# Loading the first piece of a weight in two halves, and one product of zeros fewer ahead of it

## What is computed

```python
# attention: for each token t
y[:, :, t] = einsum('bhd,bhde->bhe', rt, state + u*kt (x) vt)
state = w * state + kt (x) vt
# first feed-forward part: x (3072, 384), w1 and w2 (384, 1024), w3 (1024, 1024), w_out (1024, 384)
a = x @ w1
b = x @ w2
h = a * b @ w3
x = h @ w_out
# second: w_in (384, 2048), w_out (2048, 384)
h = x @ w_in
out = (h * cos(h)) @ w_out
```

## Time and profile before

| | us |
|---|---|
| median of 3 runs (lowest to highest) | 791.63 (791.34 to 792.43) |
| the profiled execution's own time | 792.66 |
| its span, from the first to the last record | 791.2 |
| TensorE busy, matmuls | 784.6 (99%) |
| VectorE busy | 429.4 (54%) |
| ScalarE busy | 376.4 (48%) |
| GpSimd busy | 345.8 (44%) |

### The profile page before, as it was taken

One profiled execution on the slowest core, in us unless ns is written; L12 is line 12 of the kernel. 1 busy time (PEld: TensorE's weight loads), 2 busy tenths in 40 slices (PEclk: granted clock), 3 DMA queues, 4 the chain that ended last, 5 costly groups with the idle time before them and its releaser, 6 DMA issues.

```text
span 791.2 us, 15799 instructions
## 1 busy us (share of the span) xinstructions
PE 784.6 (99%) x6500; PEld 677.2 (86%) x6500; DVE 429.4 (54%) x639; ACT 376.4 (48%) x647; POOL 345.8 (44%) x279
## 2 busy tenths in 40 slices
PE   8999999999999999999999999999999999999998
PEld 6999999888999888998888888888888888888886
DVE  7998655543644433123289555546555554554553
ACT  4634222222222222224367667656665765665664
POOL 2646766556566553111234335334333432433432
PEclk9999999999999999999999999999999999999999
DMA  8775445342344320202221010000001001001001
GB/s 335 267 244 149 114 145 152 91 137 85 105 139 144 89 88 22 80 0 73 68 80 41 2 41 0 1 8 33 1 1 40 1 1 40 1 1 39 2 1 40
DMA packets 47595, 57.32 MB, mean 72 GB/s; under 512 B 21794, under 2 KB 34211, under 8 KB 47523
## 3 DMA queue, kind: packets, MB, share of 16 engines
q1 hardware_dynamic: 34898, 45.83, 17.9%
q10 hardware_dynamic: 12624, 10.49, 4.3%
HBM read 46.86 MB, written 9.44 MB: 71 GB/s over the span
## 4 chain that ended last, share of the span: by engine, by line
PE 96%; DVE 3%; issue 1%; ACT 0%; POOL 0%; DVEq 0%; POOLq 0%
PE p_h L1164 25%; PE p_acc L1164 13%; PE p_a L1164 13%; PE p_b L1164 13%; PE p_out L1385 8%; PE p_out L1381 8%; PE p_out L1382 8%; PE p_s L1188 2%; PE p_y L1200 1%; PE p_y L1204 1%; PE p_acc L1313 1%; PE p_kv L1192 1%; DVE w3t_l L982 1%; PE p_b L1320 0%; PE p_acc L1299 0%
## 5 line engine op out<-in xcount | busy, mean ns | idle before, releaser
L626 POOL TENSOR_TENSOR g_l<-g,g_h 128x512 fp32r<-128x512 f32 x96 | 149.9, 1561 | 241.6 <-ACT g_h L814 241.6
L1113 DVE TENSOR_TENSOR g<-angle,p_h 128x512 f32<-128x512 f32 x96 | 65.8, 686 | 109.1 <-ACT angle L823 109.1
L490 POOL TENSOR_TENSOR g_l<-g,g_h 128x384 fp32r<-128x384 f32 (+1 forms) x56 | 70.2, 1253 | 121.0 <-ACT g_h L663 121.0
L1381 PE MATMUL p_out<-g_h,wq_l 128*128 128x512 f32 x288 | 112.1, 389 | 0.0
L1164 PE MATMUL p_h<-y_l,wi_h 128*128 128x512 f32 x288 | 112.1, 389 | 0.0
L1164 PE MATMUL p_h<-y_h,wi_h 128*128 128x512 f32 x288 | 112.1, 389 | 0.0
L1164 PE MATMUL p_h<-y_h,wi_l 128*128 128x512 f32 x288 | 112.1, 389 | 0.0
L1382 PE MATMUL p_out<-g_h,wq_h 128*128 128x512 f32 x288 | 112.0, 389 | 0.0
L814 ACT CAST g_h<-g 128x512 fp32r<-128x512 f32 x96 | 59.7, 621 | 67.5 <-PE p_out L1385 42.3
L658 ACT COPY g<-p_a 128x384 f32<-128x384 f32 (+1 forms) x56 | 29.4, 526 | 119.1 <-PE p_a L1164 117.5
L819 ACT ACTIVATE angle<-angle 128x512 f32<-128x512 f32 x96 | 60.6, 631 | 49.6 <-DVE angle L1123 49.6
(11 more groups left out here) (118 smaller groups left out, 1642.2 us busy)
## 6 DMA issues: line engine op xcount, KB each, us to landing
krT_raw<-in_kr_dims SPq DMA_DIRECT2D x24, 512.0 KB, 4.1
kr_raw<-in_kr_tokens SPq DMA_DIRECT2D x24, 384.0 KB, 4.7
v_raw<-in_v_tokens SPq DMA_DIRECT2D x24, 192.0 KB, 4.8
x_raw<-y_transposed SPq DMA_DIRECT2D x24, 192.0 KB, 2.5
out<-out_sb SPq DMA_DIRECT2D x17, 256.0 KB, 2.0
stage_b<-in_moe_w_in SPq DMA_DIRECT2D x8, 384.0 KB, 3.1
stage_b<-in_moe_w_out SPq DMA_DIRECT2D x8, 384.0 KB, 3.0
y_transposed<-yT ACTq DMA_DIRECT2D x24, 96.0 KB, 2.6
```

The costliest lines, as they stand in the source:

```text
L490: nc.gpsimd.tensor_tensor(g1_l[:, n % 2, cols], g1[:, n % 2, cols], g1_h[:, n % 2, cols].bitcast(F32), ALU.subtract).then_inc(s_gl, 1)
L626: nc.gpsimd.tensor_tensor(g2_l[:, par, :], g2[:, par, :], g2_h[:, par, :].bitcast(F32), ALU.subtract).then_inc(s_g2l, 1)
L1113: nc.vector.tensor_tensor(g2[:, n % 2, :], angle[:, n % 2, :], p_h[n % 4][:, :], ALU.mult).then_inc(s_g2, 1)
L1381: mm(bank[t][:, :], wq_l[:, f, cols], g2_h[:, f % 2, :], start=f == 0, stop=False)
```

## The change

`WARM` goes from 4 to 3. The load of the first piece of w_out becomes two transfers of 128 rows (192 KB) each: the first signals a new semaphore `s_row0`, the second the piece's old one, `s_st[0]`. Both are issued where the one was, so ScalarE's queue has one transfer more to issue. TensorE's product (0, 0) waits for `s_row0` alone, product (0, 1) for `s_st[0]`; ScalarE's copy of the first piece waits for both. The same bytes are loaded to the same place, and no product of real operands is added or taken away.

```diff
-WARM = 4
+WARM = 3
...
+    s_row0 = sem("first_128_rows_of_w_out_loaded")
...
+        def start_first_piece():
+
+            place = staged(A_SLOTS, 0, wo_st[0])
+            act.dma_start(place[:, 0, :], wo_st[0][:, 0, :]).then_inc(s_row0, 16)
+            act.dma_start(place[:, 1, :], wo_st[0][:, 1, :]).then_inc(s_st[0], 16)
+
         def piece(i):
 
             act.wait_ge(s_st[i % 4], 16 * (i // 4 + 1))
+            if i == 0:
+                act.wait_ge(s_row0, 16)
...
         start_w3_half(0, 0)
-        start_piece(0)
+        start_first_piece()
         start_w3_half(1, 0)
...
-            if t % 2 == 0:
+            if t == 0:
+                pe.wait_ge(s_row0, 16)
+            elif t == 1 or t % 2 == 0:
                 pe.wait_ge(s_st[t // 2], 16)
```

## The result

| | before | after |
|---|---|---|
| median of 20 executions (lowest to highest), us | 792.17 (791.34 to 793.43) | 794.22 (791.88 to 796.40) |
| ratio after / before | | 1.0022 [1.0014, 1.003] |
| the profiled execution, its span, us | 792.66, 791.2 | 794.52, 793.0 |

The kernel became slower: the medians are 2.05 us apart, and the ratio, an estimate of its own and not the quotient of the medians, says 0.22%, which is 1.7 us (the forecast was 0.34 us faster). Its executions scatter over 4.5 us where those of before scatter over 2.1. Five of the 20 took 792.4 us or less, as long as before. The profiled one is a typical one. Of 93 executions of before timed later, beside the experiments, 92 lie between 790.91 and 794.30 us, and one, with a granted clock of 0.56, took 1313.74.

A forecast was written before the change was run, and what follows sets the result against it. The prediction took TensorE's queue, with little waiting, as the bound. Its sum was -0.335 us at the fifth record, +0 issue, +0 waits, -0 lost behind: 791.63 - 0.34 = 791.3 us, range 790.2 to 792.8.

The forecast's parts named there:

- Three products of zeros, the first 128 rows on their own: TensorE's head: zeros end at 4.79 us, first half lands at 4.64, first real product starts at 4.98 instead of 5.65.
- late half: Rival at the first piece's load: both halves land together at about 5.3 us; 791.6 us, chance 0.10.
- postponed rise: Rival at TensorE's head: a pause after the zeros delays the clock's rise to 10.10 us; 792.7 us mostly, chance 0.12.
- What the low clock is worth: TensorE's head: starting 0.67 us earlier at the low clock gains half of that, 0.335 us.
- The second half, and the queue that issues it: ScalarE's queue: the added issue delays later transfers 0.47 us but costs nothing; shorter runs cost 0 to 0.1 us.
- +0 for the issue: Term of the sum for the added transfer issue on ScalarE's queue: no cost; without cover, 0.47 us.
- Where the gain goes behind the head: VectorE's chain after the head: the 0.335 us gain passes tile 2's landing and line 898, so nothing is lost.
- Swallowed: Rival behind the head: first 17 us run 0.34 us faster but VectorE's chain doesn't move; 791.6 us, chance 0.18.

The follow-up runs named there:

- e4: The kernel before, with SP waiting for the second half of w3's tile 0 instead of piece 1, so released later; 793.03 us, ratio 1.0008.
- e9: The kernel before, with the keys' chunk 1 loaded ahead of its transposed form on SP's queue; 792.38 us, ratio 1.0001.
- e11: The kernel before, no transfer added, with ScalarE's issues from the third on held for 0.7 us; 792.71 us, ratio 1.0005.
- e1: The kernel before with three products of zeros instead of four, the first piece still whole; 792.29 us, ratio 0.9999.
- e6: The kernel before with one more transfer, of 4 KB, in second place on ScalarE's queue; 792.76 us, ratio 1.0007.
- e3: The kernel after, with SP waiting for the first half of w3's tile 1 instead of piece 1; 792.35 us, ratio 1.0003.
- e8: The kernel after, with the keys' chunk 1 loaded ahead of its transposed form on SP's queue; 793.20 us, ratio 1.0013.
- e2: The kernel after with four products of zeros again, the first piece still in two halves; 792.98 us, ratio 1.0012.

## Why the prediction was wrong

**Three products of zeros, the first 128 rows on their own: right, and too cautious.** The zeros ended at 4.79 as computed. The first half landed at the lower end given, 4.47, so the first product started at 4.79 and not 4.98, and there was no gap. The late half and the postponed rise did not occur.

**What the low clock is worth: right rule, and a size that hung on the moment of the rise.** The advance was 0.86 us, half of it 0.43; the clock rose at 6.75 instead of 7.19, and half of those 0.44 us are 0.22 more. Together they are the 0.65 us at the fifth record. The ninth record (8.36 us) then waited for piece 1, landed at 8.31, and lost 0.12, which leaves 0.53 at the third piece (11.48 against 12.01) where 0.335 was forecast. The 0.22 can't be credited to the change: the moment of the rise moves by 1 us between before, e4 and e9, with the same TensorE work.

**"The second half, and the queue that issues it": this step failed.** It is the term "+0 for the issue" of the sum. It put the added issue at nothing and the shorter runs at 0 to 0.1 us, and argued that the landing of piece 1's neighbour hangs on bytes and not on the issue. Measured were 1.17 us on piece 1. By e11 a late issue alone is worth 0.47 at most, about what e1 shows without one, and in e6's one trace 4 KB more went with over a microsecond. The bytes were the same; that a transfer more changes how the others run was in no row of before. Worse, the step listed who waits for piece 1 on TensorE, and used SP's issue at 7.16 merely as a clock for the landing. SP's wait on that piece, with the attention's loads and tiles 2 and 3 behind it, was never priced. The cover of piece 1 was given as the ninth record at 8.65; on SP it was zero. e3, which moves that wait to an earlier landing, takes the loss away; it releases SP at 6.01, so it removes more than the 1.17 us.

**"Where the gain goes behind the head": right places, wrong sign.** The step named tile 2's landing with 0.3 us of cover and line 898 with 0.47, and asked whether a gain would pass. Both covers hang on SP's queue. Turned the other way they are what a delay of over 1 us runs into: 0.7 us at line 982 (17.54 to 18.26), then line 898. "Swallowed" was a rival without loss; the loss through the same two places should have been the rival on the slower side, in place of the postponed rise. e1 is the swallowed case itself: the first burst of attention products 0.5 us earlier (16.76 against 17.27), median unchanged.

**The base.** The forecast of 791.3 us stands on the median of three executions, 791.63; that of twenty is 792.17. This 0.54 us of error is the sample's and not the mechanism's. From 792.17 the same sum gives 791.8 us, still faster than before where after is slower.

**How the 2.36 us at tile 7 divide.** Only in part. The head's gain doesn't count against it: ScalarE took the first sum at 15.55 instead of 16.08 and then waited 1.15 us for tile 2. VectorE was 0.72 us behind at line 991, 1.31 at `rT_sc` ahead of line 907, and 2.27 at line 907, so the wait for GpSimd's product is the last 0.96 of it. The late release of SP alone accounts for some 0.5 by e4. The rest goes with transfers that land later than in e4 although SP issued the first of them at the same time: tile 2 (17.16 against 16.30) and the keys' chunk 1, at 22.2 us, where e4 and e6, with SP as late, had it at 19.73 and 19.85. Of that chunk's 16 parts 14 had landed by 20.16 us, the last two at 21.80 and 22.16. A fetch of instructions of 16 KB ran from 20.71 to 21.67; it can't be the reason everywhere, since in e3, where the last part of the chunk landed at 21.06 and the others by 19.47, the fetch began at 20.79 and was still running. That this lateness matters is made likely by e8, whose interval overlaps that of after; that it comes in some executions and not in others fits the five fast ones of after; what decides it stays open. e3's chunk was late with SP early, so it isn't SP's lateness alone. The difference between after (1.0022) and e2 (1.0012) is not settled either.

## What to carry to other kernels

Before adding a transfer to a queue, list every wait on every engine that hangs on the transfers issued after it, those of the queues that issue other loads first, and price each by its own slack. When a gain is bounded by some cover behind it, ask also what happens if that place comes later: the same cover bounds the loss. And time many executions: here the loss shows as scatter as much as in the median.

## What the runs showed of the hardware

A transfer more among the first few, of 192 KB or of 4 KB, went with a landing some 1 us late at unchanged bytes (plus 4 KB in e6), in seven of eight profiles. The longest packet of 1.5 to 3 KB between 3 and 9 us took 0.87 to 1.95 us in these eight and 0.66 to 1.09 in the five without; the two ranges overlap, so a single long packet doesn't tell the two kinds apart.

The moment at which the clock rises belongs to the execution. From the spacing of records it came 5.12 us after the first zeros in before, 4.08 in e4 and 4.45 in e9, whose TensorE work up to then is that of before. In the other profiles without a pause ahead of the rise it came 4.68 us (the kernel after), 3.76 (e2) and 3.3 (e8) behind the first zeros; in e11, which paused for 0.16 and 0.13 us, 6.1. The Trainium skill ("TensorE: Matmul & The Clock Gate", section "Part 1: The HAM clock gate (the "warmup" mystery)") allows 0.5 us to either side; the six profiles without a pause spread over 1.8 us, so the measurement decides. Since a moment at the low clock costs half of itself, that is up to an estimated 0.9 us of scatter in the head, more than the whole effect that was forecast.
